# Attention and a Sinkhorn-routed mixture of experts on one core: on-chip buffers begin 224 or 256 bytes further on

## The reference

```python
scores = scale * q @ k.T                  # masked to 0 <= i - j < 64, then softmax
x = (softmax(scores) @ v) as [2304, 512]
logits = x @ w_gate; P = exp(logits - logits.max())
for _ in range(8):
    P /= P.sum(1) + 1e-9; P /= P.sum(0) + 1e-9; P *= N / E
for e in range(8):                        # w1: 512 x 1024, w2: 1024 x 512
    out += P[:, e] * (relu(x @ w1[e]) @ w2[e])
```

## The kernel before, in words

| buffers | start of the first | start mod 256 |
|---|---|---|
| `x_raw`, `xv_hi`, `xv_lo`, `t_raw`, `w1_raw`, `w1_hi`, `w1_lo`, `w2_raw`, `us`, `wg` | 1,152 | 128 in all |
| `col_part`, `max_part`, `max_all` | 171,648 | 128, 160, 192 |
| `ones`, `const_sb` | 171,744 | 224 in both |
| `w2_hi0`, `w2_lo0` | 173,664 | 96 in both |
| `qk_buf`, `v_win`, `sc`, `probs`, `p_t` of the attention | 181,856 | 96 in all |
| `h_hi0`, `h_lo0`, `h_hi1`, `h_lo1`, `w2_hi1`, `w2_lo1` (in the same room, later) | 181,856 | 96 in all |

## Time and profile before

### The profile page before, as it was taken

The page is one execution under the profiler, slowest core; times in us unless marked ns, Lnnn a source line. Parts: engine busy times, 40 slices in busy tenths (PEclk is TensorE's granted clock), DMA queues, the critical chain, the costliest instruction groups (busy, mean ns, idle before and its releaser), DMA issues.

```text
span 1588.0 us, 24065 instructions
## 1 busy us (share of the span) xinstructions
PE 1576.2 (99%) x8892; PEld 1424.6 (90%) x8892; DVE 693.7 (44%) x1262; ACT 544.0 (34%) x785; POOL 991.6 (62%) x642
## 2 busy tenths in 40 slices
PE   8999999999999999999999999999999999999999
PEld 7889989999999989999999999998999999999998
DVE  7835453443443443434434434434344344344343
ACT  5742333232333333232333333243333333232331
POOL 6976565655656875655656565877656565655652
PEclk9999999999999999999999999999999999999999
DMA  8522121212121213212121221213121211212111
GB/s 251 162 75 75 59 79 54 80 54 79 53 79 55 77 53 120 80 54 79 53 79 55 77 70 62 79 53 119 54 80 55 78 69 63 79 53 79 53 66 40
DMA packets 34159, 120.44 MB, mean 76 GB/s; under 512 B 3904, under 2 KB 4160, under 8 KB 34112
## 3 DMA queue, kind: packets, MB, share of 16 engines
q1 hardware_dynamic: 34112, 119.80, 21.9%
HBM read 115.06 MB, written 4.72 MB: 75 GB/s over the span
## 4 chain that ended last, share of the span: by engine, by line
PE 92%; POOL 5%; DVE 1%; issue 1%; ACT 1%; DVEq 0%; POOLq 0%; ACTq 0%
PE ps L504 16%; PE ps L502 16%; PE ps L503 16%; PE ps L465 14%; PE ps L463 14%; PE ps L461 14%; POOL probs L852 2%; POOL xv_lo L838 1%; POOL w_lo L810 1%; POOL sc L844 1%; PE ps L353 0%; POOL w_lo L817 0%; POOL w_raw L844 0%; PE ps L409 0%; PE ps L376 0%
## 5 line engine op out<-in xcount | busy, mean ns | idle before, releaser
L810 POOL TENSOR_TENSOR w_lo<-w_raw,w_hi 128x1792 fp32r<-128x1792 f32 (+2 forms) x97 | 387.1, 3991 | 532.3 <-ACT w_hi L587 532.3
L642 ACT ACTIVATE h_hi<-ps 128x384 fp32r<-128x384 f32 x384 | 186.5, 492 | 867.6 <-DVE ps L992 430.0
L504 PE MATMUL ps<-w_hi,h_lo 128*128 128x512 f32 x1152 | 451.2, 392 | 0.0
L502 PE MATMUL ps<-w_hi,h_hi 128*128 128x512 f32 x1152 | 448.7, 390 | 0.0
L465 PE MATMUL ps<-xv_hi,w_lo 128*128 128x384 f32 x1330 | 448.2, 337 | 0.0
L503 PE MATMUL ps<-w_lo,h_hi 128*128 128x512 f32 x1152 | 448.2, 389 | 0.0
L461 PE MATMUL ps<-xv_hi,w_hi 128*128 128x384 f32 x1330 | 445.2, 335 | 1.0 <-DVE h_lo L966 0.7
L463 PE MATMUL ps<-xv_lo,w_hi 128*128 128x384 f32 x1330 | 445.8, 335 | 0.0
L966 DVE SCALAR_TENSOR_TENSOR h_lo<-ps,h_hi 128x384 fp32r<-128x384 f32 x384 | 205.8, 555 | 270.1 <-ACT h_hi L642 261.3
L463 PEld LDWEIGHTS ps<-xv_lo,w_hi 128*128 128x128 f32 x1330 | 249.6, 188 | 17.5
L461 PEld LDWEIGHTS ps<-xv_hi,w_hi 128*128 128x128 f32 x1330 | 249.7, 188 | 17.3 <-DVE h_lo L966 2.4
(11 more groups left out here) (98 smaller groups left out, 961.2 us busy)
## 6 DMA issues: line engine op xcount, KB each, us to landing
w_raw<-w SPq DMA_DIRECT2D x192, 512.0 KB, 4.0
qk_buf<-qk SPq DMA_DIRECT2D x16, 576.0 KB, 6.4
v_win<-v SPq DMA_DIRECT2D x16, 288.0 KB, 4.9
out<-x_raw SPq DMA_DIRECT2D x18, 256.0 KB, 4.4
const_sb<-consts SPq DMA_DIRECT2D x1, 176.0 KB, 3.4
wg<-w_gate SPq DMA_DIRECT2D x1, 64.0 KB, 6.5
```

The costliest lines, as they stand in the source:

```text
L502: nc.tensor.matmul(ps_y[t], h_hi[slot][:, f, c], w2_hi[slot][:, f, :], start=opens, stop=False)
L504: last = nc.tensor.matmul(ps_y[t], h_lo[slot][:, f, c], w2_hi[slot][:, f, :], start=False, stop=closes)
L642: nc.scalar.activation(h_hi[slot][:, f, half * HT:(half + 1) * HT], o, ACT.Relu)\
L810: last = nc.gpsimd.tensor_tensor(w1_lo[:, slot, c], w1_raw[:, slot, (lo + 1) * BLK:(hi + 1) * BLK], w1_hi[:, slot, c].bitcast(F32), ALU.su ...
```

## The change

`col_part`, `max_part` and `max_all` (32 bytes each, after rounding) and a new unused buffer `front` of 128 bytes are taken ahead of `x_raw`: everything from `x_raw` to `wg` begins 224 bytes further on. Behind `wg` the three are gone and so `ones` and `const_sb` begin 128 bytes further on; a new unused buffer `middle` of 128 bytes follows them, and everything from `w2_hi0` begins 256 bytes further on. Nothing reads or writes `front` or `middle`. No instruction is added, removed or put in another place.

| buffers | start mod 256 before | after |
|---|---|---|
| `x_raw` to `wg` | 128 | 96 |
| `ones`, `const_sb` | 224 | 96 |
| `w2_hi0` and all behind it | 96 | 96 |
| `col_part` | 128 | 128 |

```diff
         def sb(stack, name, shape, dt=F32):
             return stack.enter_context(nc.sbuf_tensor(name, shape, dt))
 
+
+        col_part = sb(ctx, "col_part", [P, E])
+        max_part = sb(ctx, "max_part", [P, 1])
+        max_all = sb(ctx, "max_all", [P, 1])
+        front = sb(ctx, "front", [P, 32])
 
         x_raw = sb(ctx, "x_raw", [P, SB, KT, TOKS])
 ...
         wg = sb(ctx, "wg", [P, KT, GC])
-        col_part = sb(ctx, "col_part", [P, E])
-        max_part = sb(ctx, "max_part", [P, 1])
-        max_all = sb(ctx, "max_all", [P, 1])
         ones = sb(ctx, "ones", [P, P])
         const_sb = sb(ctx, "const_sb", [P, WINDOW + 2 * P + GC])
+        middle = sb(ctx, "middle", [P, 32])
         w2_hi = [sb(ctx, "w2_hi0", [P, 2, DM], F32R)]
```

## The result

| | before | after |
|---|---|---|
| median | 1590.61 us (1589.77 to 1591.39, 6 runs) | 1597.88 us (1597.20 to 1599.47, 6 runs) |
| ratio of after to before | | 1.0048, 95% interval 1.0039 to 1.0058 |
| span of the profiled execution | 1588.0 us | 1595.4 us |

The change makes the kernel 7.3 us slower, by 0.5%. The forecast was no change, and the time lies above its range.

The account below looks back on a forecast made before the run. PE's matmul issue was taken to bound the kernel. The profiled 1589.8 us plus 0 for matmuls, other engines and transfers stayed 1589.8, stated as 1590.4 us for a median of runs, range 1588.2 to 1592.8.

Parts of the forecast that it names:

- What bounds the kernel: Whole kernel: PE is busy 99% of the span, and issuing 42 and 36 matmuls makes up a 15.52 us expert window.
- The matmuls: 4038 matmuls reading xv and w1 go from 128 to 96: taken as 0, bounds -4.0 to +4.0 us.
- The natural experiment in the trace: Matmuls of the first layer at 128 and second layer at 96 compared: 14 ns left over columns in both.
- The bound of 1 ns for a matmul: What the rows leave open for each xv and w1 matmul: -1 to +1 ns, 4.0 us over 4038.
- The range: Whole kernel time: 1588.2 to 1592.8 us, half of the matmuls' bound each way, given as -2.2 and +2.4.
- the two signs of being wrong: 384-column matmuls move off 174 ns by 1 ns or more; or windows keep 15.52 us and PE gets a several-us wait.
- Slower: PE streams or loads less smoothly from the new places: Rival at the 4038 xv and w1 matmuls: 1 ns each, 4.0 us, giving 1594.5 us and up; chance 0.05.
- Faster: what the two families of starts cost each other goes away: Rival in all 95 windows: 0.08 us each from mixed starts goes, 7.6 us, down to 1582.8; chance 0.06.
- The shortest and the median duration are equal to 1 ns: Within a run of one matmul kind: used with evenly spaced starts as evidence against the faster rival.
- The other engines: POOL, ACT and DVE on moved buffers: 63 us of bare POOL work, taken as 0, bounds -0.2 to +0.1 us.
- the transfers: 192 loads of w1 and w2: 0, since a w1 load lands in 7.3 us at worst, read after 14.6.
- the small buffers: ones, const_sb, col_part, max_part, max_all, front and middle: moving them costs 0.

Follow-up runs that it names:

- e2: Against the kernel before, everything from x_raw on moved 224 bytes further, putting x and w1 at 96, w2 and h at 64: 1590.89 us, ratio 1.0005.
- e10: Whole kernel before, with xv kept at 128 and w1, h and w2 moved to 160 modulo 256: 1585.75 us, ratio 0.9973.
- e9: PE alone, zero operands, a whole window's matmul order at many buffer distances, no kernel change: 15520 ns a window in the layout before, 15607 in the change's.
- e5: PE alone, zero operands, the kernel's matmul pattern at ten distances, then single moves and runs alone: a group of 18 takes 3.473 us at 0, 3.458 at 224.

## Why the prediction was wrong, point by point

**What bounds the kernel: right.** PE's issue sets the window, and the whole change is in it: 83 windows that are 0.087 us longer make 7.2 us, and the medians differ by 7.3.

**The matmuls: wrong, and this is the step that failed.** The prediction said: "A start at 96 therefore costs a matmul nothing that a start at 128 doesn't." Taken by itself that is so, and e2 shows it: with x and w1 at 96 the time stays. But a matmul's operand was priced by its own start, as if it were read alone. PE loads the weights of the next matmul while it streams this one's columns (PEld is busy for 89% of the span beside PE's 99%), and what counts is the distance between buffers that are read at one time. Between the two layers that distance was 224 in every window of before, and there was no row for 0. The natural experiment in the trace held the start fixed and left the neighbour out. The bound of 1 ns for a matmul was drawn around the wrong quantity: over all 78 matmuls of a window the loss is 87 / 78 = 1.1 ns. The second layer's 36, where the prediction had no unknown at all, lose 96 ns a window (2.7 ns each), and the 42 that it did price gain 10. So the term of 0 for the matmuls was 7.3 us.

**The range** took in only half of that bound. The whole of it, 1594.4 us, would have missed too, since it covered only the matmuls of the first layer. The upper end also doesn't add up: half of 4.0 and 0.1 are 2.1 us, and it has 2.4.

**The signs.** Neither of the two signs of being wrong came true. The 384-column matmuls stay within 1 ns of 174 (2.08 / 12), and PE has no new wait. The windows grew through the 512-column ones. For these the list had only what would be seen if it was right, eighteen in 4.09 us, and they took 4.12.

**The rivals.** "Slower: PE streams or loads less smoothly from the new places" named the right engine, with 1594.5 us and up, and had 0.05; it put the loss on the matmuls of xv and w1 and on their own place. "Faster: what the two families of starts cost each other goes away" came closest to the mechanism. It put the 0.08 us that a window has over 15.44 where PE changes from one kind of matmul to the other, which is where it is. It then assumed that equal starts cost nothing, and they cost more than those of before: 167 ns over 15.44 at distance 0, 80 at 224, 27 in e10. Of the eight distances of h and w2 in e9 with w1 at 0, only 128 is worse than 0.

**A row that hid it.** "The shortest and the median duration are equal to 1 ns" was read as even spacing. The excess of before was in one matmul in six to twelve: 235 ns for the last of a run of the second layer and 182 for the third behind it. A median doesn't show that, and the row's own maximum is not an issue distance. The starts in order do. The sum hid it as well: 42 x 174 + 36 x 227 = 15.48 was set against 15.52 with "so nothing else is in it", though 174 is an average over a run of twelve that holds part of the excess, and 40 ns were still missing.

**The other engines, the transfers, the small buffers at 0: right.** POOL's and ACT's pairs agree within 4 ns, the median landing went from 4.0 to 3.9 us, POOL's work at the turn takes 16.6 us as before, and the first window begins at 96.1 us of the span, where it was 96.4. By the rule of the Trainium skill that was weighed there ("DMA: Bandwidth & Descriptors", section "How a descriptor splits into AXI transactions"), the landing would be 1% shorter at most, an estimate. The medians are too coarse to say, and nobody waits for it.

## What to carry to other kernels

Where PE never idles, compare the starts of successive matmuls, position by position, and take the excess over columns plus the constant as a cost that the layout of the buffers may set. Shift whole families of operands against each other by 32 bytes with unused buffers; a kernel with PE alone and zero operands ranks the layouts, and here it gave all six windows to the nanosecond. Take its time from one matmul to the same one a period later, inside one layout. Keep the weights and the streamed operand of one run at a distance that the single run bears (0 here for h and w2), then look at the changes between runs.

## What the runs showed of the hardware

- With TensorE alone at the 2.4 GHz level, float32r, 128 x 128 weights loaded for each matmul, a matmul starts every 173.3 ns for 384 columns and 226.7 for 512 when nothing is lost: the columns and 32 ticks (e5: 72 matmuls alone take 12.484 and 16.329 us).
- The distance modulo 256 bytes between buffers loaded and streamed at one time moves this by 6 ns a matmul in a steady run of 512 columns, and for a single matmul by 12 ns in the changed kernel (185 against 173) and by up to 28 in e9 (255 against 227, with w1 at 32 and h and w2 at 96). In a steady run of 512 columns six took 1.363 us at distance 0 and 1.399 at 32; in one of 384, 1.040 at 0 and 32, 1.056 at 128. Moving everything by 224 or by 256 bytes changes nothing that can be measured (ratios 1.0005 and 0.9999).
- After a change of run the loss may last for nine matmuls (the run of eighteen after the change). Why the reads meet as they do (what in the memory is shared, and why 32 bytes matter) no run here shows.
- The Trainium skill, "SBUF — State Buffer", section "Who interferes with whom", gives PE two independent read ports for SBUF, one for the streamed operand and one for the weight load, and says that "PE and ACT never wait on anyone". In e5 no other engine reads or writes while PE works, and PE still loses 36 ns in six matmuls by the distance of those two operands. The measurement decides: for float32r, how the two operands lie to each other sets PE's pace, so its two reads are not independent in their effect.
